# Hand-staged attention and feed-forward kernel on one core: key grams of the first pass partly in other banks, query grams and state sums by parity, value scaling on GpSimd

## The reference, cut to what matters

```python
# 1. delta-rule attention: 4 batches x 8 heads, 768 steps, head_dim 48
for t in range(S):
    y[t] = q[t] @ state
    state = state + beta[t] * outer(k_n[t], v[t] - k_n[t] @ state)
# 2. feed-forward, w_in 384x2048 and w_out 2048x384, 3072 tokens
h = x @ w_in;  g = maximum(0.01 * h, h);  x2 = g @ w_out
# 3. eight experts, top 1 by x2 @ w_gate + modality_bias
out[token] = gate * (relu(x2[token] @ w1[e]) @ w2[e])
```

## Time and profile before

| | us |
|---|---|
| median of 3 runs | 981.32 |
| runs, lowest to highest | 974.87 to 982.77 |
| the profiled execution | 978.93 |
| its span from first to last instruction | 977.2 |
| PE busy | 870.9 (89%) |
| DVE busy | 553.5 (57%) |
| ACT busy | 350.6 (36%) |
| POOL busy | 87.6 (9%) |

### The profile page before, as it was taken

How to read it: one execution, slowest core, us unless ns; L and a number is a source line. 1 busy time by engine, 2 the same in 40 slices (tenths; PEclk the granted TensorE clock), 3 DMA queues, 4 the chain that set the end, 5 groups by cost and what they waited for, 6 DMA issues and landing times.

```text
span 977.2 us, 26906 instructions
## 1 busy us (share of the span) xinstructions
PE 870.9 (89%) x10528; PEld 766.0 (78%) x10529; DVE 553.5 (57%) x1578; ACT 350.6 (36%) x609; POOL 87.6 (9%) x100
## 2 busy tenths in 40 slices
PE   3775889989999998999989999999969999999962
PEld 3664678878888887888878888888759898889862
DVE  4974994588638862798359842344642333333350
ACT  3364335542545253444444342323411212121230
POOL 1000000000020002000100001010121212121210
PEclk9965899999999999999999999999999999999996
DMA  9904272345143533344153313255051111111122
GB/s 127 337 4 75 62 150 68 68 107 101 34 92 74 104 62 52 99 86 81 41 102 84 74 28 84 58 94 175 32 171 33 48 32 48 32 48 32 40 74 73
DMA packets 148308, 77.92 MB, mean 80 GB/s; under 512 B 112496, under 2 KB 144240, under 8 KB 147824
## 3 DMA queue, kind: packets, MB, share of 16 engines
q1 hardware_dynamic: 143264, 66.59, 30.4%
q0 software_dynamic: 4096, 9.48, 3.2%
...
## 4 chain that ended last, share of the span: by engine, by line
PE 67%; DVE 15%; ACT 7%; DMA 4%; issue 3%; SPq 1%; ACTq 1%; DVEq 0%; POOL 0%; POOLq 0%
PE bank L518 17%; PE bank L503 14%; PE bank L605 11%; PE bank L580 10%; DVE inv_t L1299 2%; DVE inv_tmp L1293 2%; PE bank L590 2%; PE bank L381 2%; PE bank L410 2%; ACT diag L987 2%; DVE g_raw L1368 1%; PE bank L484 1%; DVE tr L1305 1%; PE bank L471 1%; DVE inv_a L1255 1%
## 5 line engine op out<-in xcount | busy, mean ns | idle before, releaser
L518 PE MATMUL bank<-wo_hi,g_hi 128*128 128x392 f32 x384 | 139.1, 362 | 7.3 <-DVE g_lo L1373 4.0
L518 PE MATMUL bank<-wo_hi,g_lo 128*128 128x392 f32 x384 | 132.2, 344 | 0.0
L518 PE MATMUL bank<-wo_lo,g_hi 128*128 128x392 f32 x384 | 132.1, 344 | 0.0
L1368 DVE SCALAR_TENSOR_TENSOR g_raw<-g_raw 128x512 f32<-128x512 f32 x96 | 66.3, 691 | 105.0 <-ACT g_raw L1043 105.0
L503 PE MATMUL bank<-x_hi,wi_hi 128*128 128x512 f32 x288 | 118.3, 411 | 6.2 <-ACT g_raw L1043 3.4
L1043 ACT ACTIVATE g_raw<-bank 128x512 f32<-128x512 f32 x96 | 57.3, 597 | 170.5 <-PE bank L503 170.1
L503 PE MATMUL bank<-x_hi,wi_lo 128*128 128x512 f32 x288 | 114.0, 396 | 0.0
L503 PE MATMUL bank<-x_lo,wi_hi 128*128 128x512 f32 x288 | 113.9, 395 | 0.0
L1050 ACT ACTIVATE g_hi<-g_raw 128x512 fp32r<-128x512 f32 x96 | 60.7, 632 | 116.9 <-DVE g_raw L1368 116.9
L1373 DVE TENSOR_TENSOR g_lo<-g_raw,g_hi 128x512 fp32r<-128x512 f32 x96 | 66.3, 691 | 41.9 <-ACT g_hi L1050 41.7
L518 PEld LDWEIGHTS bank<-wo_hi,g_hi 128*128 128x128 f32 x384 | 72.7, 189 | 13.8 <-issue 6.0
...
## 6 DMA issues: line engine op xcount, KB each, us to landing
...
```

What stands on the lines that cost most here:

```text
L518: mm = pe.matmul(acc[i][:, 0:DX], g[f % 2][:, P * i:P * i + P], w, start=(f == 0 and k == 0), stop=(f == FT - 1 and k == 2))
L1368: dve.scalar_tensor_tensor(out=g_raw[f % 2][:], in0=g_raw[f % 2][:], scalar=0.01, in1=g_raw[f % 2][:], op0=ALU.mult, op1=ALU.max).then_inc ...
```

## The change

- `Turns` gets four more places (banks 1 to 4, numbers 3 to 6). Eight steps of the first pass are put there by name: the key gram of chunk 1 of set 0, the outputs of chunk 0 of set 0, and both key grams of set 1. `gate_weights`, the key gram of set 1 and the first `down` get waits for these banks.
- In pass -2 ACT and DVE copy out the diagonals of both chunks first; the rest of all four banks is copied by ACT afterwards. `betas` and the copy of its result move behind the grams.
- In pass -1 `outputs` of chunk 0 moves from slot 10 to slot 8, the key transposes of set 1 wholly to slot 9, `split_wi` on ACT to slots 4 (three pieces) and 7 (three), and on DVE to slots 5 to 9. DVE copies three of the four key grams of set 1, ACT one. DVE's `split_x(0)` stands ahead of the state additions.
- In every pass: `gram_q` makes a whole chunk into two banks, by even and odd pairs, at slot 15 and at the start of slot 0 (before: four pieces in slots 15, 0, 1, 2); `state_sum` likewise. The matmuls are as many as before, in another order. The odd bank has its two halves of partitions exchanged, so that `mask_q` and `add_s` take two instructions of 64 partitions for it: three for two banks.
- In every pass: all four query transposes stand in slot 13, the additions of chunk 1 to the state (`add_s(·, 1, ·)`) ahead of `norm`, and `scale_v` is done by POOL, in a loop with its clearing of `inv_t`.

```diff
...
+PLACED = {("KK", 0, 1, 0): 5, ("KK", 0, 1, 1): 6, ("Y", 0, 0, 0): 5, ("Y", 0, 0, 1): 6,
+          ("KK", 1, 0, 0): 3, ("KK", 1, 0, 1): 4, ("KK", 1, 1, 0): 5, ("KK", 1, 1, 1): 6}
...
-        self.n, self.of = 0, {}
+        self.n, self.uses, self.of = 0, [0] * 7, {}
     def take(self, step):
-        b, before = self.n % 3, self.n // 3
-        self.n += 1
+        if step in PLACED:
+            b = PLACED[step]
+        else:
+            b, self.n = self.n % 3, self.n + 1
+        before = self.uses[b]
+        self.uses[b] += 1
         self.of[step] = (b, before + 1)
...
+        att = bank[5:8] + bank[1:5]
...
         pe.wait_ge(*is_drained(("KT", t, m)))
+    if t == 1 and c == 0:
+        pe.wait_ge(s.wx_rdy, 1)
...
-def gram_q(t, m):
-    for i in range(2):
-        pe.wait_ge(*is_drained(("QT", t, m % 2 * 2 + i)))
-    b, done = fill(("QK", t, m))
+def gram_q(t, c):
+    for m in range(4):
+        pe.wait_ge(*is_drained(("QT", t, m)))
+    to = [fill(("QK", t, c, odd)) for odd in range(2)]
     for j in range(8):
-        pair = m % 2 * 8 + j
-        for hh in range(2):
-            mm = pe.matmul(b[half_p(hh), CH * j:CH * j + CH], k_t[head_p(hh), pair, chunk(m // 2)],
-                           q_t[head_p(hh), pair, chunk(m // 2)], start=True, stop=True)
-    mm.then_inc(done, 1)
+        for odd in range(2):
+            for hh in range(2):
+                mm = pe.matmul(to[odd][0][half_p(hh ^ odd), CH * j:CH * j + CH], k_t[head_p(hh), 2 * j + odd, chunk(c)],
+                               q_t[head_p(hh), 2 * j + odd, chunk(c)], start=True, stop=True)
+            if j == 7:
+                mm.then_inc(to[odd][1], 1)
...
-def state_sum(t, c, m):
-    if c == 0 and m == 0:
+def state_sum(t, c):
+    if c == 0:
...
-    b, done = fill(("S", t, c, m))
+    to = [fill(("S", t, c, odd)) for odd in range(2)]
     for j in range(8):
-        g = 16 * c + 8 * m + j
-        for hh in range(2):
-            mm = pe.matmul(b[head_p(hh), HD * j:HD * j + HD], k_raw[half_p(hh), g, :], u_sb[half_p(hh), g, :],
-                           start=True, stop=True)
-    mm.then_inc(done, 1)
+        for odd in range(2):
+            g = PAIRS * c + 2 * j + odd
+            for hh in range(2):
+                mm = pe.matmul(to[odd][0][head_p(hh ^ odd), HD * j:HD * j + HD], k_raw[half_p(hh), g, :], u_sb[half_p(hh), g, :],
+                               start=True, stop=True)
+            if j == 7:
+                mm.then_inc(to[odd][1], 1)
...
+    for odd in range(2):
+        pe.wait_ge(*is_drained(("KK", 0, 1, odd)))
...
 def slot(n, f):
     cur, nxt, ff = is_set(n + 1), is_set(n + 2), n >= 0
+    if cur and f == 0:
+        gram_q(n + 1, 1)
...
     if cur:
-        if f < 3:
-            gram_q(n + 1, f + 1)
...
-        if f == 10:
+        if f == (8 if n < 0 else 10):
             outputs(n + 1, 0)
-            if n < 0:
-                outputs(n + 1, 1)
+        if f == 10 and n < 0:
+            outputs(n + 1, 1)
...
         if f == 12:
-            state_sum(n + 1, 1, 0)
+            state_sum(n + 1, 1)
...
-        if f == 14:
-            queries_t(n + 2, 2)
-            queries_t(n + 2, 3)
         if f == 15:
             gram_q(n + 2, 0)
...
+            state_sum(n + 1, 0)
     if nxt:
-        if f == 8:
+        if f == (9 if n < 0 else 8):
             keys_t(n + 2, 0)
             keys_t(n + 2, 1)
         if f == 9:
             keys_t(n + 2, 2)
             keys_t(n + 2, 3)
-            if n == -2:
-                betas()
...
+            if n == -2:
+                betas()
+        if f == 13:
+            queries_t(n + 2, 2)
+            queries_t(n + 2, 3)
...
-for t in range(1, SETS):
-    pool.wait_ge(s.tt_ready, t)
-    pool.memset(inv_t[:], 0.0).then_inc(s.tm_zero, 1)
-    if t == 2:
+def scale_v(t):
+    pool.wait_ge(s.v_in, 128 * t + 128)
+    pool.wait_ge(s.den_rdy, t + 1)
+    pool.tensor_tensor(vals[:], vals[:], den_s[:].unsqueeze(2).broadcast_to([P, GROUPS, HD]), ALU.mult
+                       ).then_inc(s.vals_rdy, 1)
+for n in range(-1, TT - 1):
+    scale_v(n + 1)
+    if is_set(n + 2):
+        pool.wait_ge(s.tt_ready, n + 2)
+        pool.memset(inv_t[:], 0.0).then_inc(s.tm_zero, 1)
+    if n == 1:
         pool.wait_ge(s.list_out, 16)
-    if t >= 2:
-        scatter_ids(t - 2)
+    if n >= 1:
...
-        if f == 10:
+        if f == 7 and n < 0:
+            for p in range(3, 2 * KT):
+                split_wi(p)
+        if f == (8 if n < 0 else 10):
             copy_y(n + 1, 0, 0)
             copy_y(n + 1, 0, 1)
-            if n < 0:
-                copy_y(n + 1, 1, 0)
-                copy_y(n + 1, 1, 1)
-                begin_x()
         if f == 11 and n >= 0:
             copy_y(n + 1, 1, 0)
...
         if f == 10:
-            copy_gram(n + 2, 0, 0)
+            if n == -2:
+                diag_of_gram(0, 0, 0).then_inc(s.diag_a, 1)
+            elif n == -1:
+                copy_y(0, 1, 0)
+                copy_y(0, 1, 1)
+                begin_x()
+            else:
+                copy_gram(n + 2, 0, 0)
         if f == 11:
-            copy_gram(n + 2, 1, 0)
+            if n == -2:
+                diag_of_gram(0, 1, 0).then_inc(s.diag_a, 1)
+                rest_of_first_gram(0)
+            else:
+                copy_gram(n + 2, 1, 0)
         if f == 12:
             if n == -1:
                 split_x(0)
             roots(n + 2)
+            if n == -2:
+                rest_of_first_gram(1)
         if f == 13:
             copy_t(q_t, "QT", n + 2, 0)
             copy_t(q_t, "QT", n + 2, 1)
-        if f == 14:
             copy_t(q_t, "QT", n + 2, 2)
             copy_t(q_t, "QT", n + 2, 3)
     if n == -1 and f == 4:
         gate_weights()
-    if n == -1 and 5 <= f < 5 + 2 * KT:
-        split_wi(f - 5)
+        for p in range(3):
+            split_wi(p)
...
-dve.wait_ge(s.beta_tp, 1)
-dve.tensor_copy(beta_col[:], bank[0][:, 0:NC_CH * PAIRS]).then_inc(s.beta_cp, 1)
-dve.wait_ge(s.beta_cp, 1)
...
+    if t == 0:
+        dve.wait_ge(s.diag_a, 2)
+        dve.wait_ge(s.diag_d, 2)
+    else:
+        for c in range(2):
+            for odd in range(2):
+                dve.wait_ge(*is_drained(("KK", t, c, odd)))
     dve.transpose(inv_a[:], diag[:].rearrange("p g j -> p j g")).then_inc(s.gram_t, 1)
+    if t == 0:
+        dve.wait_ge(s.beta_tp, 1)
+        dve.tensor_copy(beta_col[:], bank[0][:, 0:NC_CH * PAIRS]).then_inc(s.beta_cp, 1)
+        dve.wait_ge(s.beta_cp, 1)
...
-def mask_q(t, m):
-    dve.wait_ge(*is_filled(("QK", t, m)))
-    dve.tensor_tensor(qk_t[:, eight(m), :], by_8(att_bank(("QK", t, m))[:]),
-                      mask[:].unsqueeze(1).broadcast_to([P, 8, CH]), ALU.mult).then_inc(drain(("QK", t, m)), 1)
-def scale_v(t):
-    dve.wait_ge(s.v_in, 128 * t + 128)
-    dve.wait_ge(s.den_rdy, t + 1)
-    dve.tensor_tensor(vals[:], vals[:], den_s[:].unsqueeze(2).broadcast_to([P, GROUPS, HD]), ALU.mult
-                      ).then_inc(s.vals_rdy, 1)
+def halves(odd):
+    return [(half_p(hh), half_p(1 - hh)) for hh in range(2)] if odd else [(slice(0, P), slice(0, P))]
+def mask_q(t, c, odd):
+    dve.wait_ge(*is_filled(("QK", t, c, odd)))
+    for to, at in halves(odd):
+        mm = dve.tensor_tensor(qk_t[to, every_other(c, odd), :], by_8(att_bank(("QK", t, c, odd))[at, :]),
+                               mask[at, :].unsqueeze(1).broadcast_to([to.stop - to.start, 8, CH]), ALU.mult)
+    mm.then_inc(drain(("QK", t, c, odd)), 1)
...
-def add_s(t, c, m):
-    dve.wait_ge(*is_filled(("S", t, c, m)))
-    old, new = (state[i][:, eight(m), :].rearrange("p a b -> p (a b)") for i in (c, 1 - c))
-    dve.tensor_tensor(new, old, att_bank(("S", t, c, m))[:, 0:8 * HD], ALU.add).then_inc(drain(("S", t, c, m)), 1)
+def add_s(t, c, odd):
+    dve.wait_ge(*is_filled(("S", t, c, odd)))
+    old, new = state[c], state[1 - c]
+    for to, at in halves(odd):
+        mm = dve.tensor_tensor(new[to, odd::2, :], old[to, odd::2, :], by_48(att_bank(("S", t, c, odd))[at, :]), ALU.add)
+    mm.then_inc(drain(("S", t, c, odd)), 1)
...
-        if f < 3:
-            mask_q(n + 1, f + 1)
+        if f == 0:
+            mask_q(n + 1, 1, 0)
+            mask_q(n + 1, 1, 1)
...
     if nxt and f == 15:
-        mask_q(n + 2, 0)
+        mask_q(n + 2, 0, 0)
+        mask_q(n + 2, 0, 1)
...
             copy_x(n + 1, 1)
-            scale_v(n + 1)
...
-    if nxt:
-        if f == 10:
-            copy_gram(n + 2, 0, 1)
-        if f == 11:
-            copy_gram(n + 2, 1, 1)
-        if f == 12:
-            if n == -1:
-                split_x(0)
-            norm(n + 2)
     if cur and f == 12:
+        if n == -1:
+            split_x(0)
         add_s(n + 1, 1, 0)
         add_s(n + 1, 1, 1)
+    if nxt:
+        if f in (10, 11):
+            if n == -2:
+                diag_of_gram(0, f - 10, 1).then_inc(s.diag_d, 1)
+            else:
+                if n == -1 and f == 10:
+                    copy_gram(1, 0, 0)
```

(16 more changed lines are left out.)

52 lines of the change are left out of this document (32 added, 20 removed).

## The result

The changed kernel takes 1001.6 us in the median of four runs (995.5 to 1003.4), the kernel before 979.5 (974.9 to 982.8): 1.0212 of before, with a 95% interval of 1.0164 to 1.0261. A second measurement beside other kernels gave 1.020 (1.0148 to 1.0251). The forecast was 980.5 with a range of 965 to 992: wrong, and on the other side of no change. The profiled execution of after took 1002.9 us with a span of 1001.1, 23.9 more than before's 977.2.

What follows compares the result with a forecast made beforehand. DVE was taken to bound the inversion and the first half of later passes, PE the second half. 978.9 - 5.6 (first pass) - 3.0 (later passes) + 9.5 + 0.8 (scaling on POOL) = 980.6, predicted as 980.5 us, range 965 to 992.

Steps and rivals of the forecast that it cites:

- The first pass, -5.6: First pass: earlier grams, outputs and x split, less two extra masks in the inversion, save 5.6 us.
- the copies of y: First pass: copies of the outputs of chunk 1 start at 77 in place of 79.82.
- the standstill of 1.65 us in the outputs: First pass, outputs of chunk 1: PE's unexplained 1.65 us standstill was taken to come back, giving 77 rather than 75.4.
- The scaling on POOL, +9.5 and +0.8: Slots 0 to 2: POOL's product costs DVE 1.9 us in each of sets 1 to 5, plus 0.8 in set 0.
- rival 2: Inversion: DVE stands still for all of a long POOL product, 3.5 us a set, 19.9 in all; 990.2 us, chance 0.27.
- The +0.8 of set 0: Set 0: the product's cost, partly absorbed by the 1.1 us that DVE waits at the mask.
- the half gets shorter by perhaps 0.3: Later passes, `norm` to transposes: the half shortens by perhaps 0.3 us despite more DVE work; set at nothing.
- the step on slack: DVE's full half of later passes: 1.8 us more work fits in 2.3 of slack.
- The state sums, -3.0: Later passes, PE's half: state sum of chunk 0 saves 0.5 us in five passes, chunk 1 0.5 in the last with attention.
- -8.6: Whole kernel without the product: 8.6 us less, from the first pass (-5.6) and the later passes (-3.0).

Runs made afterwards that it cites:

- a6: a5 with state sums and additions also as before, so only the first pass of the change is left: 0.9935 of before.
- a1: The changed kernel with the scaling of the values back on DVE, nothing else undone: 1.0026 of before, 992.3 us beside 990.9.
- c1: The kernel before under a second name, as control and for a profile on another chip: 1.0016 of before.
- a8: a5 with queries 2 and 3 in slot 13 as in the changed kernel: 0.9937 of before.
- a2: The changed kernel with the product still on POOL but begun later, behind the transposes of the inverse: 1.0058 of before.
- a10: a1 with the six new mask instructions spread over slots 15, 0, 1 and 2 and the second query gram in slot 1: 1.0014 of before.
- a5: a4 with query grams and masks in the four pieces and slots of before: 0.9921 of before, again 0.9904 in a second group.
- a4: a1 (scaling back on DVE) with queries 2 and 3 also back in slot 14: 1.0061 of before.
- a7: a4 with the six new mask instructions spread over slots 15, 0, 1 and 2 and the second query gram in slot 1: 1.0132 of before.
- c2: The changed kernel itself, run again on another chip beside three other runs: 1.020 of before.

## Why the prediction was wrong, point by point

**The first pass, -5.6.** Right without the new masks: a6, which has the old ones, is 6.4 us under before. Wrong for the kernel as changed, whose masks the sum of -5.6 includes. In a1, which is free of the product, the transposes of set 1 are at 137.72, against 137.59 in before and 135.85 in c1: nothing is left of the gain. `norm` of set 0 did start 3.9 us sooner. But the first mask came at 32.76 where 32.1 was forecast, since PE waited 0.99 us for the last query copy before the new gram; the three masks took 2.14 and not 2.0; the next three took 2.14 again, where three single ones take 1.8 (0.61 from start to start in a8); and the transposes of set 0 stood at 50.78, not at 49.6. Then came PE's standstill in the key grams of set 1. The hit at the copies of y (76.86 for 77) is luck in part: the inversion ended 1.9 us too late, and the standstill of 1.65 us in the outputs, which the forecast let come back, didn't.

**The scaling on POOL, +9.5 and +0.8.** This step failed in its size. The mechanism was named as rival 2, the size was set by choice at 1.9 us a set, somewhat more than the length of DVE's own product. POOL's needs 2.77 with nothing in its way and DVE loses 2.6 or 2.7. The +0.8 of set 0 held: DVE's wait at the mask (1.61 us in a1) took up all but 0.7. Measured: 17 to 18 us (a1 against after), 10.3 forecast. Rival 2 had this term at 19.9 and, with the rest of the sum, 990.2; it was the nearest of the cases and had 0.27, but it too lies 11 us under the result, and its 3.5 us a set are too long. The rule of SBUF — State Buffer in the Trainium skill (Who interferes with whom) agrees with the trace: in after, a DVE instruction with two SBUF inputs stood until the product was done in five of the six sets, and in a2 those with a PSUM input ran on at 0.69. Its GPSIMD Engine Reference (Elementwise — side-by-side cycle accounting) gave an estimate of 3.4 us for the length; here the shortest rows are 2.76 and 2.77.

**The masks, "the half gets shorter by perhaps 0.3".** The new grams and masks are the second cause: they cost 8 to 9 us (a1 and a10 against a8). But the step on slack was not the one that failed. In a later half with a granted clock of 1.00 it came out better than forecast: 45.5 us in before, 44.3 in a1. One reason is a slip in the prediction, which counts an addition to the state more in this half; two of them, 1.02 us, leave it. What the step missed is that the price falls where there is no slack, up to the transposes of set 1 (6 to 8 us between a8 and a1 or a10), and that the clock doesn't stay.

**The state sums, -3.0.** Not seen as such: a5 against a6 gives 0.14%, 1.4 us, within the intervals. The addition ahead of `norm` only moves work: in a5 the full halves of sets 3 to 5 last 43.9 us where they last 45.4 or 45.5 in a6, but the halves from transposes to `norm` sum to 237.7 against 232.2.

**The queries in slot 13.** The forecast gave them nothing. a8 against a5 gives 0.16 to 0.33%, within the intervals; they cannot be told from nothing. With the new gram and slot 14, in a4 and a7, the wait for queries is 16.9 and 16.8 us.

**The clock.** The forecast had no term for it. In the full halves of sets 3 to 5 the granted clock was 1.00 in before, c1, a5 and a6; 0.96 in one of the three in a1 and in all three in c2; 0.93, 1.00 and 0.90 in after. The same half lasts 44.3 us at 1.00 and 45.9 at 0.96 in a1, and 46.9 at 1.00, 49.3 at 0.93 and 50.8 at 0.90 in after. That is the size of what the stops alone leave open, but no run changed the clock and nothing else, so its share stays open.

By the ratios, from before: -6.4 for the first pass, -1.4 for the state sums, +8.5 for the grams and masks, +17.5 for the product make 18, where 1.020 to 1.021 are 20; the rest is within the intervals. Against the forecast, the kernel without the product is 11 us too slow (+2.6 in place of -8.6), and the product 7 us too dear (17.5 in place of 10.3).

**The version that beats both.** a5 keeps the first pass and the state sums, and leaves the scaling and the query grams as they were: 0.9904 and 0.9921 of before in two groups, 8 to 9 us less, with both intervals below 1.
